# Expert loop unrolled, output rows written at the next tile's head, idle matmuls in the routing tail

## The reference

```
do_compute = x @ w_skip > 0
out = x.copy()
e_idx = argmax(xc @ w_gate)          # xc: rows with do_compute
for e in range(8):
    h = max(xc[mask] @ w1[e], 0)     # 384 -> 1024
    y[mask] = gate_w * (h @ w2[e])   # 1024 -> 384
out[do_compute] = xc + y
```

## Time and profile before

| | |
|---|---|
| median of 3 runs | 931.82 us |
| profiled execution | 934.12 us |
| its span | 932.4 us |
| mean granted TensorE clock | 0.955 of full |
| busy: TensorE, VectorE, ScalarE, GpSimd | 86%, 70%, 54%, 45% |

### The profile page before, as it was taken

The page is one execution under the profiler, slowest core; times in us unless marked ns, Lnnn a source line. Parts: engine busy times, 40 slices in busy tenths (PEclk is TensorE's granted clock), DMA queues, the critical chain, the costliest instruction groups (busy, mean ns, idle before and its releaser), DMA issues.

```text
span 932.4 us, 27901 instructions
## 1 busy us (share of the span) xinstructions
PE 801.2 (86%) x10858; PEld 648.3 (70%) x10859; DVE 650.3 (70%) x1303; ACT 500.6 (54%) x1099; POOL 415.9 (45%) x500
## 2 busy tenths in 40 slices
PE   0314769999999999999999999999956899999986
PEld 0313648888787878787878788887735677788864
DVE  5378877887878888888888877865666825533382
ACT  4435545767576766666766666555454514412261
POOL 4314242626363635454454524343314646644463
PEclk9975698999999999999999999999986999999998
DMA  9782844676766766747575475420645833611100
GB/s 240 131 213 44 144 76 82 122 119 129 117 131 115 122 127 122 130 93 151 92 144 105 91 133 100 84 58 19 198 142 198 303 119 122 223 51 51 36 22 16
DMA packets 309830, 109.97 MB, mean 118 GB/s; under 512 B 284930, under 2 KB 301364, under 8 KB 309344
## 3 DMA queue, kind: packets, MB, share of 16 engines
q1 hardware_dynamic: 304000, 94.63, 48.9%
q0 software_dynamic: 3232, 7.64, 2.4%
q10 hardware_dynamic: 2496, 6.29, 1.9%
HBM read 60.39 MB, written 20.46 MB: 87 GB/s over the span
## 4 chain that ended last, share of the span: by engine, by line
PE 61%; DMA 11%; DVE 9%; SPq 7%; issue 4%; ACT 4%; POOL 3%; DVEq 0%; POOLq 0%; ACTq 0%
PE b_acc L681 16%; PE b_h L668 15%; PE b_ch L606 9%; PE b_acc L807 8%; PE b_h L791 7%; SPq L453 4%; DMA natq<-x_dram,id_in 3%; PE b_gr L572 3%; DMA operands<-t_dram 3%; DMA t_dram<-inv 3%; PE b_ch L572 2%; DMA natq<-in_q_dram 1%; DVE inv L1234 1%; ACT inv L826 1%; DVE inv L1228 1%
## 5 line engine op out<-in xcount | busy, mean ns | idle before, releaser
L1612 POOL TENSOR_TENSOR stage<-stage 128x256 f16<-128x256 f32 x192 | 142.4, 742 | 266.7 <-ACT stage L826 266.0
L668 PE MATMUL b_h<-stage,wt 128*128 128x256 f16 x1728 | 221.6, 274 | 5.2 <-DVE stage L1298 3.2
L681 PE MATMUL b_acc<-wt,stage 128*128 128x384 f16 x1152 | 219.4, 327 | 2.4 <-POOL stage L1612 0.4
L668 PEld LDWEIGHTS b_h<-stage,wt 128*128 128x128 f16 x1728 | 159.6, 98 | 26.1 <-DVE stage L1298 6.1
L681 PEld LDWEIGHTS b_acc<-wt,stage 128*128 128x128 f16 x1152 | 106.2, 98 | 59.7 <-POOL stage L1612 6.9
L826 ACT ACTIVATE stage<-stage 128x256 f16<-128x256 f32 x192 | 80.0, 416 | 98.7 <-DVE stage L1298 97.7
L1298 DVE SCALAR_TENSOR_TENSOR stage<-b_h,stage 128x256 f32<-128x256 f32 x192 | 80.6, 420 | 69.3 <-ACT stage L937 69.1
L807 PE MATMUL b_acc<-wt,operands 128*128 128x384 f16 x576 | 101.6, 326 | 7.0 <-DVE operands L1530 7.0
L791 PEld LDWEIGHTS b_h<-y,wt 128*128 128x128 f16 x1728 | 100.3, 99 | 8.3 <-issue 6.3
L791 PE MATMUL b_h<-y,wt 128*128 128x128 f16 x1728 | 102.9, 222 | 3.2 <-DVE y L1161 2.9
L572 PE MATMUL b_gr<-operands 128*128 128x128 f16 x576 | 44.6, 233 | 53.1 <-DMA operands<-operands 20.6
(11 more groups left out here) (174 smaller groups left out, 1269.8 us busy)
## 6 DMA issues: line engine op xcount, KB each, us to landing
operands<-in_moe_w_dram SPq DMA_DIRECT2D x16, 1536.0 KB, 7.5
a_sys<-a_dram SPq DMA_DIRECT2D x24, 256.0 KB, 4.3
natq<-in_q_dram SPq DMA_DIRECT2D x24, 192.0 KB, 3.9
raw_v<-in_v_dram SPq DMA_DIRECT2D x24, 192.0 KB, 4.1
stage<-y SPq DMA_DIRECT2D x96, 48.0 KB, 2.1
x_dram<-stage SPq DMA_DIRECT2D x24, 192.0 KB, 2.8
out_dram<-stage SPq DMA_DIRECT2D x24, 192.0 KB, 3.2
natk<-in_k_dram SPq DMA_DIRECT2D x22, 192.0 KB, 4.0
```

The lines of the kernel that those rows point to most:

```text
L668: mm = pe.matmul(b_h[f % 2][:, 0:GT], wt[0][:, a, d * FF + f * P:d * FF + (f + 1) * P], xT[:, g % 2, b, d, :], start=(i == 0), stop=(i == ...
L681: mm = pe.matmul(b_acc[w][:, 0:DM], g16[:, f % 4, a, w * P:(w + 1) * P], wt[1][:, b, f * DM:(f + 1) * DM], start=(f == 0 and (a, b) == PAR ...
L1612: pool.tensor_tensor(g16[:, f % 4, LO, :], g32[:, f % 4, :], g16[:, f % 4, HI, :], ALU.subtract).then_inc(g_lo, 1)
```

## The change

Five edits, all in the routing tail or the expert tiles:

1. `keep_going(n)` issues n matmuls of 512 columns into `b_acc[1]`, whose result nobody reads: 10 after `ranks(2)`, 24 after the list's last matmul, 4 after the first tile's transposes.
2. The loop over pairs of experts becomes straight code for 8 experts on TensorE, ScalarE and VectorE (the loop over an expert's tiles stays); TensorE's and part of ScalarE's semaphore bookkeeping at an expert's head goes.
3. ScalarE's order in a first tile becomes quarter 0, relu, quarter 1, relu, quarter 2, `tile_in`, quarter 3.
4. VectorE writes tile t-1's output rows at the head of tile t. Its order in a first tile becomes: rows of the tile before, quarter 0, hidden_low, quarter 1, hidden_low, `tile_in`, quarter 2, quarter 3. In the very first tile quarter 0 follows the first hidden_low. A last `rows_out` stands behind the loop.
5. GpSimd copies `yout` to `yleft` and scatters from there. VectorE may then write `yout` again once the copy is made, and no longer waits for the scatter before.

```diff
+            def keep_going(n):
+                for _ in range(n):
+                    pe.matmul(b_acc[1][:], before16[:], mask_p[:], start=True, stop=True)
...
             ranks(2)
+            keep_going(10)
...
             mm.then_inc(list_done, 1)
+            keep_going(24)
...
             transpose_x(0)
-            with pe.Fori(0, E // 2) as e2:
-                for i in range(2):
...
+            keep_going(4)
+            for e in range(E):
+                i = e % 2
...
+                with pe.Fori(0, n) as j:
+                    expert_tile(before + j, i, 4 * e + 4)
```

ScalarE's tile:

```diff
             def tile(t, split=None):
                 if split:
                     split_hi(*split, 0)
-                    split_hi(*split, 1)
                 relu(t, 0)
                 if split:
-                    split_hi(*split, 2)
+                    split_hi(*split, 1)
                 relu(t, 1)
                 if split:
+                    split_hi(*split, 2)
+                tile_in(t + 1)
+                if split:
                     split_hi(*split, 3)
-                tile_in(t + 1)
```

VectorE's tile:

```diff
+            def rows_out(t):
+                dve.wait_ge(ea_done, 1 + t)
+                dve.wait_ge(xg_kept, t)
+                dve.wait_ge(yo_left, t)
+                dve.scalar_tensor_tensor(yout[:], b_acc[0][:, 0:DM], xg_keep[:, DM:MR], xg_keep[:, 0:DM],
+                                         ALU.mult, ALU.add).then_inc(yo_ready, 1)
+
             def tile(t, split=None):
-                if split:
-                    split_lo(*split, 0)
+                if not isinstance(t, int):
+                    rows_out(t)
+                    if split:
+                        split_lo(*split, 0)
                 hidden_low(t, 0)
                 if split:
+                    split_lo(*split, 0 if isinstance(t, int) else 1)
+                hidden_low(t, 1)
+                if split and isinstance(t, int):
                     split_lo(*split, 1)
-                hidden_low(t, 1)
+                tile_in(t + 1)
                 if split:
                     split_lo(*split, 2)
-                tile_in(t + 1)
-                dve.wait_ge(ea_done, 1 + t + 1)
-                dve.wait_ge(xg_kept, t + 1)
-                dve.wait_ge(yo_left, 1 + t + 1)
-                dve.scalar_tensor_tensor(yout[:], b_acc[0][:, 0:DM], xg_keep[:, DM:MR], xg_keep[:, 0:DM],
-                                         ALU.mult, ALU.add).then_inc(yo_ready, 1)
-                if split:
                     split_lo(*split, 3)
...
+            rows_out(before + n)
```

GpSimd's loop:

```diff
                 pool.wait_ge(yo_scattered, 16 * t + 16)
-                pool.sem_inc(yo_left, 1)
+                waited()
                 pool.tensor_copy(id_out[:], ids[:, ds(t, 1)]).then_inc(ids_ready, 1)
                 pool.wait_ge(yo_ready, 1 + t + 1)
                 waited()
+                pool.tensor_copy(yleft[:], yout[:]).then_inc(yo_left, 1)
                 pool.wait_ge(ids_ready, 2 * t + 3)
+                waited()
+                pool.wait_ge(yo_left, 1 + t + 1)
                 waited()
                 pool.indirect_dma_start(
                     out=out, out_offset=bass.IndirectOffsetOnAxis(ap=id_out[:], axis=0),
-                    in_=yout[:], in_offset=None, bounds_check=T - 1, oob_is_err=False).then_inc(yo_scattered, 16)
+                    in_=yleft[:], in_offset=None, bounds_check=T - 1, oob_is_err=False).then_inc(yo_scattered, 16)
```

More of the change, by code:

```diff
@@ L177, in build @@
         yout = y32[:].rearrange("p b e -> p (b e)")[:, DM:2 * DM]
+        yleft = nq16[:].rearrange("p l u i -> p (l u i)").bitcast(F32)[:, 0:DM]
         xgT = y32[:].rearrange("p b e -> p (b e)")[:, 0:DM].bitcast(F16).rearrange("p (l m) -> p l m", l=2)
@@ L813, in _ @@
             transpose_x(0)
-            with pe.Fori(0, E // 2) as e2:
-                for i in range(2):
[L816 to L821, removed]
+            keep_going(4)
+            for e in range(E):
+                i = e % 2
+                n = pe.value_load(tile_n[0:1, 0, e:e + 1], min_val=1, max_val=NT)
+                before = pe.value_load(tile_n[0:1, 1, e:e + 1], min_val=e, max_val=MAXT)
+                pe.wait_ge(ew_ready, 4 * e + 2)
+                with pe.Fori(0, n) as j:
+                    expert_tile(before + j, i, 4 * e + 4)
         @block.scalar
@@ L984, in split_hi @@
                 if k == 0:
-                    act.wait_ge(w1_loaded[i], 8 * e + (16 if i == 0 else 8))
+                    act.wait_ge(w1_loaded[i], 16 * (e // 2) + 16)
                 if k == 2:
-                    act.wait_ge(w2_loaded[i], 8 * e + (16 if i == 0 else 8))
+                    act.wait_ge(w2_loaded[i], 16 * (e // 2) + 16)
                 copy(wt[i][:, HI, k * QW:(k + 1) * QW], stages[i][:, k * QW:(k + 1) * QW], W1S[k]).then_inc(ew_hi, 1)
@@ L1132, in _ @@
             tile_in(0)
[L1133 to L1137, removed]
+            for e in range(E):
+                n = act.value_load(tile_n[0:1, 0, e:e + 1], min_val=1, max_val=NT)
+                before = act.value_load(tile_n[0:1, 1, e:e + 1], min_val=e, max_val=MAXT) if e else 0
+                if e:
                     act.wait_ge(eh_done, 1 + 2 * before)
                     act.sem_inc(act_waited, 1)
[L1140 to L1149, removed]
+                tile(before, (e + 1, (e + 1) % 2) if e + 1 < E else None)
+                with act.If(n > 1):
+                    with act.Fori(1, n) as j:
+                        tile(before + j)
         @block.vector
@@ L1553, in _ @@
             split_lo(0, 0, 3)
-            with dve.Fori(0, E // 2) as e2:
-                for i in range(2):
-                    e = 2 * e2 + i
-                    n = dve.value_load(tile_n[0:1, 0, ds(e, 1)], min_val=1, max_val=NT)
-                    before = dve.value_load(tile_n[0:1, 1, ds(e, 1)], min_val=0, max_val=MAXT)
-                    if i == 0:
-                        tile(before, (e + 1, 1))
-                    else:
-                        with dve.If(e2 < E // 2 - 1):
-                            tile(before, (e + 1, 0))
-                        with dve.If(e2 >= E // 2 - 1):
-                            tile(before)
-                    with dve.If(n > 1):
-                        with dve.Fori(1, n) as j:
-                            tile(before + j)
+            for e in range(E):
+                n = dve.value_load(tile_n[0:1, 0, e:e + 1], min_val=1, max_val=NT)
+                before = dve.value_load(tile_n[0:1, 1, e:e + 1], min_val=e, max_val=MAXT) if e else 0
+                tile(before, (e + 1, (e + 1) % 2) if e + 1 < E else None)
+                with dve.If(n > 1):
+                    with dve.Fori(1, n) as j:
+                        tile(before + j)
+            rows_out(before + n)
         @block.gpsimd
```

## The result

| | before | after |
|---|---|---|
| median of 10 runs each, same session | 931.13 us (928.34 to 934.34) | 934.78 us (933.24 to 936.4) |
| ratio, 95% interval | | 1.0028 (1.0016 to 1.0041) |
| profiled execution, its span | 934.12, 932.4 us | 933.24, 931.5 us |
| busy: TensorE, VectorE, ScalarE, GpSimd | 86%, 70%, 54%, 45% | 87%, 70%, 54%, 46% |

What follows compares the result with a forecast made beforehand. Changeable time: the wait before the tiles and 15.7 us in or behind split-weight tiles, VectorE nearly full in four. Terms sum to +1.45 us on 934.12; the same step on 931.82 gives 933.3, range 930.8 to 935.8 (8 in 10: 923.5 to 938.0).

Steps and rivals of the forecast that it cites:

- The clock and the ramp: Before and in tile 0: idle matmuls raise TensorE's clock, transposes held 0.8 us, tile 1 starts earlier; minus 1.6 us.
- Tiles 1 to 3: Split tiles 1 and 2, and tile 3: GpSimd's copy and scatter wait for VectorE's quarters, delaying next rows; plus 2.4 us.
- Tiles 7 and 8: Tile 7 falls to 8.95 us (minus 0.3), tile 8 rises to 8.55 (plus 0.15) through later output rows.
- Tiles 9 and 10: Together minus 1.25 or plus 0.4 us, by whether the new copy gets in before quarter 0; taken as minus 0.4.
- the bad one: Tiles 9 and 10: new copy not in before quarter 0, tile 9 at 9.95 us, tile 10 at 9.2; plus 0.4.
- Tiles 20, 21, 22: Tile 20 minus 0.85 us, single-tile expert's tile 21 plus 0.95, tile 22 behind it plus 0.7.
- The end: End of the run: the new copy's cost shows once there, plus 0.4 us.
- Unrolling: Expert heads: saved address arithmetic and branches hidden behind quarters and tile_in; 0 us, minus 0.3 to plus 0.5.
- GpSimd keeps up: Rival: GpSimd gets copy and scatter in between quarters, VectorE bounds TensorE; minus 7.15 us, 924.7 us, chance 0.25.
- GpSimd is late at every head: Rival: quarter 0 blocks the new copy in tiles 7, 9 and 20 too; plus 5.1 us, 936.9 us, chance 0.22.
- The idle matmuls don't work: Rival: clock still half at tile 0, transposes held up to 4 us; 934.9 to 938.9 us, chance 0.10.

Runs made afterwards that it cites:

- the repeat: The changed kernel run once more with no edit, compared with the kernel before: 937.28 us, 1.0035.
- the second order: Changed kernel with GpSimd's loop reordered: natk, gather, xg_keep copy, then the previous tile's copy to yleft and scatter; 930.97 us, 0.9967 of the kernel before.
- the turns alone: Kernel before with only edit 3 and VectorE's tile_in ahead of quarter 2, output rows between quarters 2 and 3: 933.59 us, 0.9996 of before.

## Why the prediction came out right

The forecast was no change with a slight loss, by GpSimd; the result is that, inside the forecast's own range (930.8 to 935.8), on its slow side. Part of that is luck: the repeat (1.0035) would lie outside the 0.3%, and terms that were off cancelled. Step by step:

- **The clock and the ramp** (-1.6): right in mechanism. The two traces have -2.7 and -2.0. The delay of the transposes, taken as 0.8 between 0 and 4, was nothing in one (0.15 from the copy's end to their start, 705.31 to 705.46, as before) and 0.84 in the other.
- **Tiles 1 to 3** (+2.4): the chain came as worked out, quarter 0 ahead of the copy and quarter 1 ahead of the scatter. It measured +1.5 and +2.1, less than forecast: output rows began 3.67 us into tile 1 and the transposes 9.69, where the sum had 3.8 and 10.0; in tile 2 the transposes came at 9.05.
- **Tiles 7 and 8** (-0.15): mis-sized, measured +0.35. Tile 7 was right (8.83 for 8.95). For tile 8 I had output rows end 3.2 us into it, the scatter at 5.7 and the copy at 6.2. In the profile VectorE's rows end at 3.65 (785.69), the scatter at 6.25, the copy at 6.77: 0.5 late at each step from the first. Two things I had not seen: tile 7's own transposes are 0.36 late, because the new copy was held there after all, which moves `tile_in` and with it both quarters ahead of the rows; and these two quarters take 3.78 us, not 3.5, beside GpSimd's gather and its copy to `xg_keep`. How the 0.5 divides between them isn't shown.
- **Tiles 9 and 10** (-0.4): I stood between two branches; the bad one was true. The copy did not get in before quarter 0: the index copy ahead of it met the quarter (1.80 us for 0.19), the copy came behind it (0.50), and the scatter fell into quarter 1 (2.27). Tile 9 is 9.85 (9.95 in that branch), tile 10 9.15 (9.2): +0.24.
- **Tiles 20, 21, 22** (-0.85, +0.95, +0.7): -0.98, +1.17, +0.90.
- **The end** (+0.4): +0.32.
- **Unrolling** (0, at most +0.5): the term that failed. The run with it alone says +3.1 us (1.4 to 4.7), of which 0.66 is seen in the tiles behind tile 3. A shorter head was taken as hidden; it moved VectorE's first quarter ahead of the scatter.

Sum by these terms: -2.7 + 1.5 + 0.35 + 0.24 - 0.98 + 1.17 + 0.90 + 0.32 = +0.8 for the first trace; the second has +2.2. The forecast said +1.45. The ratios say +2.6 and, in the repeat, +3.3. The terms behind tile 3 alone came to +2.0 where I had +0.65, and in the first trace errors of the other sign ahead of tile 4 (-1.2 where I had +0.8) hid that.

Of the rivals, "GpSimd keeps up" fell with the rows of tile 1, and the second order shows what it was worth with GpSimd really in time: 3.4 us from the list to the end and 3.1 in the ratio, not 7.15, since tile 1 stays long and the late scatters hold tile 4. "GpSimd is late at every head" was half true: in tiles 7 and 20 its condition held (the copy was held by quarter 0, 2.12 and 2.09 us), but not its price (8.83 and 8.82 for 9.95), since the scatter got in ahead of quarter 1, which the rival, like the forecast, had not worked out; in tile 9 the price came. "The idle matmuls don't work" fell with tile 0.

**What stays open.** Why unrolling costs more in the medians than its trace shows. One profile against a median is good to about 3 us here, since the part ahead of the list alone differs by 3.1 between two executions of the changed kernel. Some 1.7 us of that are there 20 us into the run, where the same VectorE operation on the loaded queries starts at 20.00 us in one and at 21.70 in the other; four kernels that keep the loop have it at 20.00, 20.20, 21.43 and 21.79, so the change doesn't make it. The run with TensorE alone unrolled doesn't decide it. Whether fetching the code has to do with it is open too: from 680 us on the instruction queue moved 7 packets where it had moved 3 (8 with TensorE alone unrolled), and no run tells whether an engine stood for them. The prices don't add up either: edits 1 to 4 together measured 0.9987, though unrolling alone measured 1.0033 and neither the idle matmuls nor the turns alone showed a gain. Edit 4 was not run by itself. Tile 1 stayed above 11.5 us in every run that has edits 2 to 4 (11.53 without the idle matmuls, 11.83 without the copy).

## What to carry to other kernels

Where two engines share a chain, add a small operation only after looking at what the other engine does in the same microsecond: this copy takes 0.5 us alone and cost 4 us, since at the heads it started beside one of VectorE's quarters and, where the next quarter followed at once, pushed the scatter into it. Put the work that others wait for (here `natk`, the gather and `xg_keep`) ahead of work that nobody waits for (the scatter), and give the deferred work its own buffer; the buffer without the order cost 0.4% against the same kernel without it, and the order without the buffer 1.7%. And when a filled idle stretch makes one tile faster, ask what the next tile waits for; here, in the old order, it waited for quarters that stood behind GpSimd's copies, just longer.

## What the runs showed of the chip that was not expected

The clock fell behind short waits within dense work, in some executions only. The windows view of the second run of the changed kernel, tile 1 (the last three columns are TensorE's granted clock, DMA share and GB/s):

```profile
724.00:726.00 2.00, 0.00 (x0) 0.00 (x0) 2.00 (x2) 1.91 (x2) 1.83 (x1) 1.00 1.03 411
726.00:728.00 2.00, 1.68 (x8) 0.89 (x9) 2.00 (x3) 0.00 (x0) 1.04 (x2) 0.74 1.05 391
728.00:730.00 2.00, 2.00 (x9) 1.15 (x8) 0.53 (x1) 0.00 (x0) 1.78 (x3) 0.50 1.04 376
730.00:732.00 2.00, 2.00 (x13) 1.25 (x12) 0.95 (x2) 1.48 (x2) 1.09 (x2) 0.91 0.86 345
```

TensorE had stood 2.41 us, and through that wait the granted clock was full. It fell within 0.7 us of the first matmul behind it (0.95 over 726.5 to 727, 0.50, 1.2 GHz, from 727 on) and stayed at half until about 730; in the first run of the same program the same wait left it at full clock. That costs some 1.3 us (3.44 for 2.12) in executions that meet it. The second order shows it too (3.59 us behind 2.41), unrolling alone in tile 2 (3.58 behind 2.35), TensorE alone unrolled (3.80 behind 2.79) and the idle matmuls alone (3.46 behind 2.38). The length of the wait doesn't tell who meets it: the clock stayed full behind 2.23 us in the kernel before (2.13), behind 2.65 with the turns alone (2.12), and behind 3.30 without the copy (2.12).

Whether the idle matmuls find the clock up is as uncertain. The windows view of the changed kernel's first profile:

```profile
692.00:694.00 2.00, 2.00 (x6) 0.76 (x5) 1.76 (x8) 0.88 (x1) 0.00 (x0) 0.50 0.06 1
694.00:696.00 2.00, 0.87 (x3) 0.15 (x1) 1.78 (x7) 0.00 (x0) 0.00 (x0) 0.91 0.02 0
...
698.00:700.00 2.00, 1.57 (x14) 0.88 (x12) 1.04 (x7) 0.39 (x1) 0.00 (x0) 0.50 0.00 0
700.00:702.00 2.00, 2.00 (x8) 0.76 (x7) 1.64 (x1) 0.00 (x0) 1.45 (x1) 0.70 0.00 0
702.00:704.00 2.00, 2.00 (x11) 0.94 (x10) 0.12 (x1) 0.00 (x0) 1.11 (x1) 1.00 0.07 16
```

Nearly all of the ten ran at half clock (4.00 us for ten); it came up about when they ended (0.91 over 694 to 696) and was down again at 698, before the 24 began. So the ten bought the 24 nothing here: those had to raise it anew, which it did at about 701 in this run, and in the second run, where they took 7.52 us for 6.44, only after 706. No run leaves out the ten alone.
